# Products with the values in every other visit: two at a time, one copy of 512 columns for both

## The reference, cut to what matters

```python
scores = scale * np.matmul(q, k.transpose(0, 1, 3, 2))
...
keep = is_sink | in_window
scores = np.where(keep, scores, -1000000000.0)
scores = scores - np.max(scores, axis=-1, keepdims=True)
a = np.exp(scores)
a = a / (np.sum(a, axis=-1, keepdims=True) + 1e-09)
return np.matmul(a, v).astype(np.float32)
```

## Time and profile before

| | |
|---|---|
| median of 3 runs | 639.79 us (639.69 to 639.91) |
| the profiled execution | 639.95 us, span of its records 638.2 us |
| granted clock of TensorE | 0.998 of full speed |
| busy over the span | PE 97%, PEld 84%, DVE 65%, ACT 46%, POOL 43% |
| attention loop | up to about 143 us; DMA 0.73 to 0.76 busy there |

### The profile page before, as it was taken

The page is one execution under the profiler, slowest core; times in us unless marked ns, Lnnn a source line. Parts: engine busy times, 40 slices in busy tenths (PEclk is TensorE's granted clock), DMA queues, the critical chain, the costliest instruction groups (busy, mean ns, idle before and its releaser), DMA issues.

```text
span 638.2 us, 14188 instructions
## 1 busy us (share of the span) xinstructions
PE 621.8 (97%) x3984; PEld 535.6 (84%) x3984; DVE 412.7 (65%) x1026; ACT 293.8 (46%) x823; POOL 272.1 (43%) x340
## 2 busy tenths in 40 slices
PE   6999999999999999999999999999999999999995
PEld 4677777777888888888888888899899999999993
DVE  5788888887864465545744557778846647648550
ACT  6888898887523223232332323624324334334231
POOL 4876777782313113122131122455534534545420
PEclk9999999999999999999999999999999999999999
DMA  7678777764121171215311373231422021120011
GB/s 248 222 234 269 249 247 235 245 228 151 59 67 33 49 248 34 66 33 173 123 33 58 102 252 100 68 131 56 160 83 98 8 94 54 47 99 33 17 50 54
DMA packets 61337, 76.71 MB, mean 120 GB/s; under 512 B 4208, under 2 KB 41328, under 8 KB 61296
## 3 DMA queue, kind: packets, MB, share of 16 engines
q1 hardware_dynamic: 61296, 76.24, 36.9%
HBM read 51.06 MB, written 25.17 MB: 119 GB/s over the span
## 4 chain that ended last, share of the span: by engine, by line
PE 92%; POOL 2%; issue 2%; DMA 1%; SPq 1%; POOLq 0%; DVE 0%; ACT 0%; DVEq 0%
PE acc L1595 31%; PE ps_p L1647 19%; PE ps_o L1687 10%; PE ps_th L1584 10%; PE ps_y L608 6%; PE ps_s L552 6%; PE ps_t L575 3%; PE ps_t L580 2%; PE ps_x L1572 2%; PE ps_o L624 2%; DMA v_sink<-vS 1%; DMA x_res<-xT_scratch 1%; PE ps_o L628 1%; POOL g_lo L1224 0%; POOL w2l L310 0%
## 5 line engine op out<-in xcount | busy, mean ns | idle before, releaser
L1192 POOL TENSOR_TENSOR z_lo<-z_raw,z_hi 128x512 fp32r<-128x512 f32 x47 | 61.6, 1332 | 203.2 <-ACT z_hi L1276 203.2
L1595 PE MATMUL acc<-w2h,z_hi 128*128 128x512 f32 (+1 forms) x384 | 131.3, 342 | 0.0
L1595 PE MATMUL acc<-w2h,z_lo 128*128 128x512 f32 (+1 forms) x384 | 129.3, 337 | 0.0
L1595 PE MATMUL acc<-w2l,z_hi 128*128 128x512 f32 (+1 forms) x384 | 129.3, 337 | 0.0
L351 ACT ACTIVATE probs<-masked,neg_max 128x132 f32<-128x132 f32 (+1 forms) x192 | 80.2, 423 | 21.3 <-DVE neg_max L437 9.5
L1595 PEld LDWEIGHTS acc<-w2h,z_lo 128*128 128x128 f32 x384 | 72.8, 190 | 8.0
L1595 PEld LDWEIGHTS acc<-w2h,z_hi 128*128 128x128 f32 x384 | 72.8, 190 | 8.0 <-issue 0.2
L1595 PEld LDWEIGHTS acc<-w2l,z_hi 128*128 128x128 f32 x384 | 72.9, 190 | 7.7
L1394 DVE TENSOR_TENSOR xT_lo<-ps_x,xT_hi 128x512 fp32r<-128x512 f32 x24 | 16.6, 690 | 80.0 <-ACT xT_hi L1253 80.0
L1224 POOL TENSOR_TENSOR g_lo<-g_raw,g_hi 128x384 fp32r<-128x384 f32 x32 | 32.5, 1016 | 71.4 <-ACT g_hi L1332 71.4
L1507 DVE SCALAR_TENSOR_TENSOR ps_g<-m_raw,conv_w,ps_g 128x384 f32<-128x384 f32 x112 | 62.0, 619 | 0.2
(11 more groups left out here) (114 smaller groups left out, 1499.1 us busy)
## 6 DMA issues: line engine op xcount, KB each, us to landing
v_sb<-vP SPq DMA_DIRECT2D x16, 384.0 KB, 4.8
x_scratch<-x_sb SPq DMA_DIRECT2D x16, 384.0 KB, 2.7
x_nat<-x_scratch SPq DMA_DIRECT2D x24, 256.0 KB, 2.8
xT_scratch<-xT_raw SPq DMA_DIRECT2D x24, 256.0 KB, 2.2
x_res<-xT_scratch SPq DMA_DIRECT2D x24, 256.0 KB, 3.1
uT_scratch<-u_sb SPq DMA_DIRECT2D x24, 256.0 KB, 2.9
uT<-uT_scratch SPq DMA_DIRECT2D x8, 768.0 KB, 4.5
out<-o_sb SPq DMA_DIRECT2D x24, 256.0 KB, 2.0
```

The lines of the kernel that those rows point to most:

```text
L1192: nc.gpsimd.tensor_tensor(z_lo[s % ZR][:, part, :], z_raw[:, part, :], z_hi[s % ZR][:, part, :].bitcast(F32), ALU.subtract).then_inc(z_lo_ ...
L1595: last = nc.tensor.matmul(bank, l, r, start=first and s == 0 and m == 0 and a == 0, stop=s == T - 1 and m == 1 and a == 2, skip_group_chec ...
```

## The change

The bank `ps_y` is used whole: product number j of a round goes to columns 0 to 255 if j is odd and to 256 to 511 if it is even, and a *group* is two products that share the bank. Both products of a group are issued in one visit, in visits 1, 3 and 5; visits 0, 2 and 4 have none. One copy of 512 columns by ScalarE, in visits 1, 3 and 5, takes a group's y to one of three `y_sb` of 512 columns. The turns of y come one visit later than before (first the visit 0 part in a pair's visit 2, then the others in visits 0 and 1 of the pair after next), and so do both parts of `normalise`. On GpSimd `split_sinks` goes behind `w_split`. After the loop the order is adapted, and VectorE's first `mix.xT` goes behind the evacuation of the last pair. The number of matmuls stays the same. `v_sink0` and the `y_sb` get other places in memory.

```diff
+        def group(s, m):
+            j = VISITS * s + m
+            return (j + 1) // 2, slice(0, 2 * P) if j % 2 else slice(2 * P, 4 * P)
...
@@ GpSimd, step
                     values_over(n, s, it)
-                    split_sinks(n, s, it)
                     if first and s == 0:
+                        split_sinks(n, s, it)
                         for e in range(2):
                             gather_sinks(n, e)
                     for e in range(2):
                         w_split(2 * n + e, it, 2 * s + e)
                     if not (first and s == 0):
+                        split_sinks(n, s, it)
@@ ScalarE
-            def evac_y(n, m):
-                act.wait_ge(pv_done, VISITS * n + m + 1)
-                wait_count(act, y_turned, VISITS * (n - 1) + m + 1)
-                nc.scalar.copy(y_sb[m][:], ps_y[:, 0:2 * P]).then_inc(y_evac[m], 1)
+            def evac_y(it, j, halves):
+                act.wait_ge(pv_done, 2 * VISITS * it + j - 2)
+                wait_count(act, y_turned, 2 * VISITS * it + j - 6)
+                nc.scalar.copy(y_sb[(j - 3) // 2 % 3][:, halves], ps_y[:, halves]).then_inc(y_evac, 1)
...
-                        if started:
-                            evac_y(n - 1, v)
+                        if j % 2 and started:
+                            evac_y(it, j, slice(2 * P, 4 * P) if first and j == 3 else slice(0, 4 * P))
@@ VectorE, step
-                        if v == 1 and not first:
-                            normalise(n - 2, s, it - 1, False)
-                        if v == 2 and started:
-                            normalise(n - 1, 1 - s, it if s == 1 else it - 1, True)
+                        if v != 1 and not first:
+                            normalise(n - 2, s, it - 1, v == 0)
@@ VectorE, after the loop
-            evac_y(PAIRS - 1, 0)
-            mix.xT(0, 0)
+            normalise(PAIRS - 2, 0, IT - 1, True)
+            evac_last_y(0)
             evac(PAIRS - 1, VISITS - 1)
             normalise(PAIRS - 2, 0, IT - 1, False)
+            mix.xT(0, 0)
@@ TensorE, pv
-                    wait_count(pe, y_evac[VISITS - 1], n)
+                if m == 2 and isinstance(n, int) and n == PAIRS - 1:
+                    pe.wait_ge(y_last[1], 1)
                 else:
-                    pe.wait_ge(y_evac[m - 1], n + 1)
+                    wait_count(pe, y_evac, 3 * (loads - 1) + g)
@@ TensorE, step
                         qk(n, s, v, it + 1)
-                        if started:
-                            pv(n - 1, 1 - s, v, it + s)
+                        if j == 1 and not first:
+                            pv(n - 1, 1, 0, it)
+                            pv(n - 1, 1, 1, it)
+                        elif j == 3:
+                            if not first:
+                                pv(n - 2, 1, 2, it)
+                            pv(n - 1, 0, 0, it + 1)
+                        elif j == 5:
+                            pv(n - 1, 0, 1, it + 1)
+                            pv(n - 1, 0, 2, it + 1)
...
-                        if v == 0 and not first:
-                            turn_y(n - 2, s, VISITS - 1)
-                        if v > 0 and started:
-                            turn_y(n - 1, 1 - s, v - 1)
+                        if v < 2 and not first:
+                            turn_y(n - 2, s, v + 1, it)
+                        elif v == 2 and started:
+                            turn_y(n - 1, 1 - s, 0, it + s)
@@ TensorE, after the loop
-            turn_y(PAIRS - 2, 0, VISITS - 1)
+            turn_y(PAIRS - 2, 0, 1, IT)
+            turn_y(PAIRS - 2, 0, 2, IT)
+            pe.wait_ge(y_last[0], 1)
             pv(PAIRS - 1, 1, 1, IT)
```

More of the change, by code:

```diff
@@ L146, in fast_path @@
         x_sb = [place(nc, f"x_sb{s}", [P, T, P], F32, X_RES_AT + 4 * S * s) for s in range(2)]
-        y_sb = [place(nc, f"y_sb{m}", [P, 2 * P], F32, U_SB_AT + 8 * P * m) for m in range(VISITS)]
-        v_sink0 = place(nc, "v_sink0", [P, T - 2, P], F32, U_SB_AT + 8 * P * VISITS)
+        y_sb = [place(nc, f"y_sb{g}", [P, 4 * P], F32, U_SB_AT + ROW * g) for g in range(3)]
+        v_sink0 = place(nc, "v_sink0", [P, T - 2, P], F32, CHAIN_AT + 4 * ROW)
         q_sb = [early.q_sb, q_sb1]
@@ L192, in fast_path @@
         pv_done = sem("pv_done")
-        y_evac = [sem(f"y_evac{m}") for m in range(VISITS)]
+        y_evac = sem("y_evac")
+        y_last = [sem(f"y_last{m}") for m in range(VISITS)]
         y_turned = sem("y_turned")
@@ L373, in evac_sinks, with evac_last_y @@
                 nc.scalar.copy(sinkT[:], ps_t[1][:, 0, 0:P]).then_inc(sink_evac, 1)
-            def evac_y(n, m):
-                act.wait_ge(pv_done, VISITS * n + m + 1)
-                wait_count(act, y_turned, VISITS * (n - 1) + m + 1)
-                nc.scalar.copy(y_sb[m][:], ps_y[:, 0:2 * P]).then_inc(y_evac[m], 1)
+            def evac_y(it, j, halves):
+                act.wait_ge(pv_done, 2 * VISITS * it + j - 2)
+                wait_count(act, y_turned, 2 * VISITS * it + j - 6)
+                nc.scalar.copy(y_sb[(j - 3) // 2 % 3][:, halves], ps_y[:, halves]).then_inc(y_evac, 1)
+            def evac_last_y(m):
+                g, half = group(1, m)
+                act.wait_ge(pv_done, VISITS * (PAIRS - 1) + m + 1)
+                act.wait_ge(y_turned, VISITS * (PAIRS - 1) - 2)
+                nc.scalar.copy(y_sb[g % 3][:, half], ps_y[:, half]).then_inc(y_last[m], 1)
             def step(it, first=False):
@@ L404, in _ @@
             evac(PAIRS - 1, VISITS - 1)
-            evac_y(PAIRS - 1, 1)
+            evac_last_y(1)
             evac_sinks(PAIRS - 1)
@@ L410, in _ @@
             mix.sine(0, 0)
-            evac_y(PAIRS - 1, 2)
+            evac_last_y(2)
             mix.cosine(0, 0)
@@ L455, in evac, with evac_last_y @@
                                         ALU.mult).then_inc(evac_v, 1)
[L457 to L461, removed]
+            def evac_last_y(m):
+                g, half = group(1, m)
+                dve.wait_ge(pv_done, VISITS * (PAIRS - 1) + m + 1)
+                dve.wait_ge(y_turned, VISITS * (PAIRS - 1) - 4)
+                nc.vector.tensor_copy(y_sb[g % 3][:, half], ps_y[:, half]).then_inc(y_last[m], 1)
             def invert(n, s):
@@ L584, in pv @@
             def pv(n, s, m, loads):
-                k = VISITS * n + m
+                g, half = group(s, m)
                 if m == 0:
                     pe.wait_ge(v_in[s], 16 * loads)
-                    wait_count(pe, y_evac[VISITS - 1], n)
+                if m == 2 and isinstance(n, int) and n == PAIRS - 1:
+                    pe.wait_ge(y_last[1], 1)
                 else:
-                    pe.wait_ge(y_evac[m - 1], n + 1)
+                    wait_count(pe, y_evac, 3 * (loads - 1) + g)
                 pe.wait_ge(evac_a, 4 * n + 2 + m)
@@ L607, in pv, with turn_y @@
                         keysT = probsT[:, e].rearrange("p t k -> p (t k)")[:, src:src + width]
-                        last = nc.tensor.matmul(ps_y[rows, dst:dst + width], values[:, rows], keysT,
+                        last = nc.tensor.matmul(ps_y[rows, half][:, dst:dst + width], values[:, rows], keysT,
                                                 start=a == 0, stop=a == len(passes) - 1, skip_group_check=True)
                 last.then_inc(pv_done, 1)
-            def turn_y(n, s, m):
+            def turn_y(n, s, m, loads):
+                g, half = group(s, m)
+                y = y_sb[g % 3][:, half]
                 if m < 2:
                     wait_count(pe, normed, 2 * n + m)
-                pe.wait_ge(y_evac[m], n + 1)
+                if isinstance(n, int) and n == PAIRS - 1:
+                    pe.wait_ge(y_last[m], 1)
+                else:
+                    pe.wait_ge(y_evac, 3 * (loads - 1) + g + 1)
                 if m > 0:
@@ L624, in turn_y @@
                     last = nc.tensor.matmul(ps_o[:, (first + t) * P:(first + t + 1) * P],
-                                            y_sb[m][:, t * P:(t + 1) * P], ident[:], start=t == 0,
+                                            y[:, t * P:(t + 1) * P], ident[:], start=t == 0,
                                             stop=m == 0, is_transpose=True, skip_group_check=True)
@@ L671, in _ @@
             pv(PAIRS - 1, 1, 2, IT)
-            turn_y(PAIRS - 1, 1, 1)
-            turn_y(PAIRS - 1, 1, 2)
+            turn_y(PAIRS - 1, 1, 1, IT)
+            turn_y(PAIRS - 1, 1, 2, IT)
             mix.theta(0, 2)
```

4 lines of the change are left out of this document (3 added, 1 removed).

## The result

The changed kernel takes 645.63 us (median of 4 runs, 644.75 to 646.51) where the kernel before takes 639.74 (639.68 to 639.91): ratio 1.0096, 95% interval 1.0084 to 1.0108. It is slower, as forecast (645.1, range 642.0 to 648.5). The profiled execution took 644.75 us, its span is 643.1, at a granted clock of 0.998.

A forecast was written before the change was run, and what follows sets the result against it. TensorE was taken as the bound, VectorE's chain barely hidden. A round: 17.68 - 0.45 + 0.84 + 0.18 + 0.45 = 18.70 against 17.78; loop +5.15 and tail +0.2 on 639.79 gave 645.1 us, range 642 to 648.5.

The forecast's parts named there:

- Visits 2 to 3, stall 0.84: Attention loop: VectorE's chain needs 2.90 + 0.69 = 3.59, TensorE's own work takes 2.75, so TensorE stalls 0.84 a round.
- Visits 0 to 1, stall 0.45: Attention loop: TensorE's work 2.87 against VectorE's 3.14, plus 0.18 for masks late behind evacuation and moved `normalise`; stall 0.45.
- Visits 4 to 5, stall 0.18: Attention loop: TensorE's own work 3.41 against 3.59 for VectorE's chain of maxima, so a stall of 0.18 a round.
- part 2: ScalarE's larger copies of y wait for the double product, making exponentials slightly late: zero, with 0.1 a visit as bound.
- Joins, 0.15 each: TensorE's double products in visits 1, 3, 5: each join saves 0.15 of start and step, 0.45 a round; bounds 0 and 0.60.
- Copies on ScalarE: Six 256-column copies of y become three of 512: 0.41 of duration goes, worth nothing by itself since ScalarE sits idle.
- Values of odd pairs: Odd pairs' values load a visit later; issue to `values_over` should fall from 5.40 to under 4, so it fits.
- rival C: Much slower: GpSimd's gather of sinks decides the round, at least 14.3 plus load time, up to 19.7; 651 us; chance 0.10.
- Start and end: Outside the steady rounds: start unchanged, tail to the last sinks' turn +0.2, between -0.7 and +0.8.
- part 4: VectorE's moved `normalise` costs zero, bound 0.1; a pair's store leaves SP's queue a visit later, also zero.
- Rival A: Faster: TensorE stays the bound in every visit and the joins gain 3.0, giving 636.8 us; chance 0.10.
- Rival B: No measurable change: stalls and joins cancel, as if maxima came 0.3 earlier in each visit; about 640 us; chance 0.10.

The follow-up runs named there:

- e5: Changed kernel with VectorE's merges left out, so its output lacks the merge of shared and own columns: 641.35 us, ratio 1.0031.
- e1: Changed kernel with one product issued in every visit again, the rest of the change kept: 639.70 us, ratio 0.9997 to the kernel before.
- e3: Changed kernel with late turns of y moved to visits 0 and 4 and the odd pair's third product to visit 2: 638.87 us.
- e9: Changed kernel with the first `normalise` moved to the end of the visit before, its turn of y ahead of the probabilities' turn: 644.86 us.
- e4: Changed kernel with ScalarE's copy of y behind all four exponentials in visits 1, 3 and 5: 645.14 us, ratio 1.0083.
- e10: e7 with the first `normalise` moved to the end of the visit before, its turn of y ahead of the probabilities' turn: 638.81 us.
- e12: e3 with the first two loads of x ahead of the store of pair 13 in SP's queue: 637.95 us, ratio 0.9977.
- e7: e3 with TensorE's turn of the first tile of x put later behind the loop: 638.60 us, ratio 0.9985.

## Why the prediction was right, step by step

**Visits 2 to 3, stall 0.84: right.** 3.59 forecast, 3.59 measured, and the cause is shown by e5 (chain shortened), e1 and e3 (product put back). A chain that was hidden needs no new row: both halves of 3.59 were in the trace of before, 2.90 in the pair's own visit and 0.69 at the only place where TensorE really waited.

**Visits 0 to 1, stall 0.45: right in size,** 98.81 - 95.48 = 3.33 against 2.87, so 0.46. The last maximum came 98.12 - 95.48 = 2.64 after the scores, 0.19 later than the 2.45 of before, where the prediction took 0.18. (Its own working gives 1.8 - 1.57 = 0.23 for the first mask, and not the 0.26 that it says; measured are 1.06 against 0.77, so 0.29.) e9 shows that moving the `normalise` away gives back 0.11; as the evacuation came 0.22 later there, its full share is not shown.

**Visits 4 to 5, stall 0.18: right in size by luck, wrong in cause.** 111.48 - 107.92 = 3.56, so 0.15. But it was the bound of part 2 ("0.1 a visit") and not the maxima: the copy of y, held by the double product, made ScalarE late for the sinks' turn. I had added up VectorE's chain alone where two chains end within 0.1 of each other; e4 shows the second behind the first.

**Joins, 0.15 each: right.** Two products take 106.99 - 105.32 = 1.67, where one of 0.80 and one of 1.02 make 1.82; in visit 5 it is 1.90 for 2.04. The Trainium skill ("TensorEngine Tiling (Array Packing)", key properties) has a change of tiling mode drain the engine. The trace agrees so far as a join, which has one change fewer, saved 0.15; that the drain is what costs it no run shows. The round then adds up: 17.69 (e1) - 0.44 + 0.84 + 0.46 + 0.15 = 18.70.

**Copies on ScalarE.** ScalarE's groups over 39 to 137 us of the changed kernel, to set against the earlier trace rows:

```profile
L358 ACT ACTIVATE probs<-masked,neg_max 128x132 f32<-128x132 f32 (+2 forms) x126 | 52.1, 415 | 12.7 <-DVE neg_max L452 12.4 <-PE ps_t L590 0.3
...
L386 ACT COPY y_sb<-ps_y 128x512 f32<-128x512 f32 x16 | 9.3, 579 | 2.0 <-PE ps_y L624 1.6
```

A copy of 512 columns took 0.579, so (2 x 0.359 - 0.579) x 3 = 0.42 a round was saved, 0.41 forecast. The 0.9 that the budget of the Trainium skill gave ("ScalarE: Activation LUTs", rules for kernel authors) is not borne out; the page gives that budget for an ACTIVATE whose bias is a pointer operand, and the prediction laid it on copies. Either was worth nothing, as said: the exponentials wait for maxima, 12.4 us in all, and e1, which keeps the large copies, gains nothing by them.

**Values of odd pairs: right.** `values_over` of the odd pair starts 109.60 - 106.45 = 3.15 after its load's issue ("under 4"), and in the five rounds no exponential waited for `gathered`, so rival C is out in the changed kernel. Its mechanism is real, though: in e3, e10 and e12, with rounds about 1 us shorter, the gather came late in one or two rounds of five.

**Start and end.** The start came at 26.85 (27.06 before), as forecast unchanged within the scatter. The tail is the term that was mis-sized: +0.62 where I took +0.2, inside my bounds (e1, with 8.16 for 7.58, had it too). I had followed VectorE's and TensorE's order there but not SP's, though part 4 says that the store leaves a visit later; behind the last such store stands the load of x. The sum of the profiled execution: +5.18 in the loop, -0.21 at its start, +0.62 in the tail, -0.69 behind it (487.13 against 487.82), -0.10 around the span, together 4.80 = 644.75 - 639.95. The -0.69 has no cause in this change that I could find, and the spans of the four runs differ by 1.9 us; the median stands 0.9 above the profiled execution. So that 645.1 came this near to 645.63 is in part luck; what the working got right is the loop, +5.18 where it has +5.15.

**Rival A** is out: scores of visit 3 start 2.04 after those of visit 2, but run 1.55 to the next stage. My picture of "idle before the scores" was wrong in form: nearly no idle time is shown, the rows of the scores are longer. The second product started 106.24 - 105.32 = 0.92 after the first (forecast 0.87 to 0.9), and VectorE was idle for 0.85 before the evacuation in visit 5, as forecast. **Rival B** (maxima 0.3 earlier) is out by the time itself, and e5 says why: even 0.66 earlier, where there are merges, leaves 641.35 (e5).

## What to carry to other kernels

An engine that is shown busy for 97% of the time may just be hiding a chain of another engine that is nearly as long as its own work (here 2.90 against 3.02). Before work is bunched, add up for each stage the time from its start to the answer that the next one needs, and compare it with what is left in between; what is saved by joining (0.15) is small against one uncovered chain (0.84). Leave a stage without its usual work only where something else can fill it: products two, one, one, two, with the turns of y in the bare visits, beat both kernels, though by 0.7 us only (1.4 with the earlier load of x). And follow each moved step into the queues that it issues to: the last store of a loop can hold the first load of the next stage.

## What was not expected of the hardware

A stall of TensorE between matmuls of one row shows as a longer row (1.62 for 0.93) and not as idle time: a busy share of 99.5% (18.61 of 18.70) held 1.45 us of waiting. From VectorE's last maximum to the stage of TensorE behind the scores that had waited for it, it took 0.69 us in the changed kernel, in e3 and in e5 alike. The same load of values at the same place in SP's queue reached its user after 5.10 us in a round of e7 and 5.98 in one of e10.
